# The second expert product in quarters of the output columns, each combined and stored while the next one is made, and half a weight place loaded a tile sooner

## What is computed

```python
h = x @ w_in                                   # 3072 x 2048
g = (a0 + a1*h + a2*h**2 + a3*h**3) / (1 + |b0|*|h| + |b1|*h**2 + 1e-6)
x = g @ w_out                                  # 3072 x 512

logits = x @ phi                               # 3072 x 32
d = softmax(logits, over the tokens)
slot_input = d.T @ x                           # 8 experts x 4 slots x 512
for e in range(8):
    h = np.maximum(slot_input[e] @ w1[e], 0.0) # 4 x 1024
    slot_out[e] = h @ w2[e]                    # 4 x 512
c = softmax(logits, over the slots)
out = c @ slot_out                             # 3072 x 512
```

## Time and profile before

| | |
|---|---|
| median of 3 runs | 519.40 us (519.39 to 519.45) |
| profiled execution | 519.27 us, span 517.5 us |
| busy share of the span: PE, DVE, ACT | 97%, 85%, 77% |
| DMA | 85.3 MB, of it 6.29 MB written |
| chain that ended last | PE 92%, ACT 2%, DMA 2%, DVE 1% |

### The profile page before, as it was taken

How to read it: one execution, slowest core, us unless ns; L and a number is a source line. 1 busy time by engine, 2 the same in 40 slices (tenths; PEclk the granted TensorE clock), 3 DMA queues, 4 the chain that set the end, 5 groups by cost and what they waited for, 6 DMA issues and landing times.

```text
span 517.5 us, 15763 instructions
## 1 busy us (share of the span) xinstructions
PE 503.0 (97%) x6568; PEld 380.1 (73%) x6568; DVE 441.0 (85%) x821; ACT 399.0 (77%) x776; POOL 0.2 (0%) x4
## 2 busy tenths in 40 slices
PE   8899999999999999999999999999999999999993
PEld 7667777877787787778778777877877787654552
DVE  4898999999999999999999999999999999951133
ACT  2877989888888988888898888889888988921122
POOL 0000000000000000000000000000000000000000
PEclk9999999999999999999999999999999999999997
DMA  8982275366313122311313232131322214999998
GB/s 343 418 355 98 90 267 196 95 243 229 119 64 105 42 91 75 97 51 63 104 44 93 72 80 68 63 104 44 100 66 72 75 43 141 424 420 408 417 365 348
DMA packets 18934, 85.29 MB, mean 165 GB/s; under 512 B 2096, under 2 KB 2224, under 8 KB 13488
## 3 DMA queue, kind: packets, MB, share of 16 engines
q1 hardware_dynamic: 18720, 84.09, 44.2%
q10 hardware_dynamic: 144, 0.20, 0.1%
HBM read 77.99 MB, written 6.29 MB: 163 GB/s over the span
## 4 chain that ended last, share of the span: by engine, by line
PE 92%; ACT 2%; DMA 2%; DVE 1%; issue 1%; SPq 0%; DVEq 0%; ACTq 0%
PE hb L425 17%; PE hb L427 17%; PE hb L426 17%; PE gb L355 10%; PE sl L472 4%; PE at L355 4%; PE mb L449 4%; PE at L402 4%; PE at L378 3%; DMA g<-w_in 2%; PE at L615 1%; PE hb L615 1%; PE hb L652 1%; PE mb L457 1%; PE mb L355 1%; PE hb L361 1%
## 5 line engine op out<-in xcount | busy, mean ns | idle before, releaser
L425 PE MATMUL hb<-w_hi,x_hi 128*128 128x512 f32 x384 | 160.2, 417 | 0.8 <-DVE x_lo L955 0.8
L427 PE MATMUL hb<-w_hi,x_lo 128*128 128x512 f32 x384 | 151.7, 395 | 0.0
L426 PE MATMUL hb<-w_lo,x_hi 128*128 128x512 f32 x384 | 151.4, 394 | 0.0
L742 ACT ACTIVATE hs<-hb 128x512 f32<-128x512 f32 x96 | 57.2, 596 | 44.3 <-PE hb L427 44.3
L427 PEld LDWEIGHTS hb<-w_hi,x_lo 128*128 128x128 f32 x384 | 72.1, 188 | 17.7
L425 PEld LDWEIGHTS hb<-w_hi,x_hi 128*128 128x128 f32 x384 | 72.2, 188 | 15.0 <-issue 2.0
L426 PEld LDWEIGHTS hb<-w_lo,x_hi 128*128 128x128 f32 x384 | 72.4, 189 | 12.9
L964 DVE SCALAR_TENSOR_TENSOR h<-h,few,ab 128x512 f32<-128x512 f32 x96 | 71.9, 749 | 10.2 <-ACT h L746 9.9
L751 ACT ACTIVATE h<-h,few 128x512 f32<-128x512 f32 x96 | 70.1, 730 | 9.1 <-DVE h L964 9.1
L969 DVE SCALAR_TENSOR_TENSOR tt<-tt,cst,hs 128x512 f32<-128x512 f32 x96 | 72.2, 752 | 3.4
L979 DVE SCALAR_TENSOR_TENSOR g<-tt,cst,h 128x512 f32<-128x512 f32 x96 | 71.4, 746 | 2.3 <-ACT h L755 0.2
(11 more groups left out here) (154 smaller groups left out, 540.4 us busy)
## 6 DMA issues: line engine op xcount, KB each, us to landing
place<-w SPq DMA_DIRECT2D x27, 1024.0 KB, 9.6
v_in<-v_windows SPq DMA_DIRECT2D x24, 520.0 KB, 3.7
kw<-k_windows SPq DMA_DIRECT2D x24, 512.0 KB, 4.6
qT<-q_t SPq DMA_DIRECT2D x24, 256.0 KB, 2.8
place<-w SPq DMA_DIRECT2D x10, 512.0 KB, 16.6
wout<-w_out_t SPq DMA_DIRECT2D x4, 1024.0 KB, 14.6
wout<-w_out SPq DMA_DIRECT2D x4, 1024.0 KB, 9.0
g<-w_in SPq DMA_DIRECT2D x3, 1024.0 KB, 10.3
```

Source lines behind the costliest of these rows:

```text
L425: mm(o, x_hi[:, p, xs], w_hi[:, f, kd, :], start=kd == 0, stop=False)
L426: mm(o, x_hi[:, p, xs], w_lo[:, f, kd, :], start=False, stop=False)
L427: i = mm(o, x_lo[:, p, xs], w_hi[:, f, kd, :], start=False, stop=kd == KD - 1)
```

## The change

The second product is cut in quarters of 128 output columns instead of halves of 256. A stage of w2 is now one quarter for one group of experts with the whole hidden dimension, 32 matmuls of 128 columns; the order of the stages is quarter 0 and 1 of the first group, 0 and 1 of the second, then quarters 2 and 3 (`W2_STAGES`). The host lays out w2 and the output accordingly. `combine(quarter, part)` makes 16 tiles (part 0: banks of four tiles, 512 columns) or 8 (part 1: banks of two tiles, 256 columns), with matmuls of 128 columns and five banks throughout. Each part has one store, of 1 MB or of 512 KB, from places `o_0` to `o_3` that lie where stages 5 to 7 of w1 were.

`x_hi` and `x_lo` become one buffer `x`, in which the two parts of a tile lie together, so that the part of the even tiles is 4 KB in one piece. The first half of a place of stage 8 is put there, and loaded when the hidden product of tile 22 is done, ahead of the w1 loads that wait for tile 23.

```diff
-        x_hi = sb("x_hi", [P, 2, KD * P], f32r)
-        x_lo = sb("x_lo", [P, 2, KD * P], f32r)
+        x = sb("x", [P, 2, 2, KD * P], f32r)
...
+        x_hi, x_lo = x[:, :, 0, :], x[:, :, 1, :]
...
-        pairs += [in_att + QB * ATT, in_g, in_tmp, in_wout, in_wout + 2 * QB, (in_tmp + 2 * QB, in_wout + 7 * QB)]
+        pairs += [(in_att + QB * ATT, in_att + QB * (ATT + 1)), in_g, in_tmp, in_wout, in_wout + 2 * QB, (in_tmp + 2 * QB, in_wout + 7 * QB)]
...
-        HC = DM // 2
+        HC = DM // 4
+        W2_STAGES = ((0, 0), (1, 0), (0, 1), (1, 1), (2, 0), (2, 1), (3, 0), (3, 1))
+        SETS = ((0, 1), (2,))
...
-        o_bank = [at[:, 0, :], at[:, 1, :], gb[:, :], at[:, 2, :], sl[:, :], hb[:, 0, :], hb[:, 1, :]]
-        o_banks = (5, 7)
+        o_banks = [at[:, 0, :], at[:, 1, :], gb[:, :], hb[:, 0, :], hb[:, 1, :]]
...
-        y_bank = [[at[:, 2, :], sl[:, :]], [hb[:, 0, :], hb[:, 1, :]]]
+        y_bank = [at[:, 2, :], sl[:, :]]
...
             load_pair(3, 1)
+            sp.wait_ge(h_psum, (N - 1) * FC)
+            load_half(8, 0)
             for f in range(FC):
                 sp.wait_ge(h_psum, (N - 1) * FC + f + 1)
                 load_pair(4 + f, 0)
                 load_pair(4 + f, 1)
-            load_pair(8, 0)
+            load_half(8, 1)
...
+            for quarter in range(4):
+                for part in range(2):
+                    cs = slice(16 * HC * part, 16 * HC + 8 * HC * part)
+                    sp.wait_ge(o_dve, 4 * quarter + 2 * part + 2)
+                    sp.wait_ge(o_act, 4 * quarter + 2 * part + 2)
+                    sp.dma_start(out[quarter, :, cs], o_place[quarter][:, cs]).then_inc(stored, 16)
...
+            def combine(quarter, part):
+                cs = slice(HC * quarter, HC * quarter + HC)
+                if part == 0:
+                    pe.wait_ge(s_kept, quarter + 1)
...
+                k = 0
+                for a in SETS[part]:
+                    for m in range(2):
+                        for r in range(4):
+                            u = o_use(quarter, part, r) - len(o_banks)
+                            if k == 0 and u >= 0:
+                                pe.wait_ge((o_dve, o_act)[u % 2], u // 2 + 1)
+                            rows = slice(NS * r, NS * r + NS)
+                            i = mm(o_bank(quarter, part, r)[:, HC * k:HC * k + HC], cT[rows, 2 * a + m, :], s_rows[rows, cs],
+                                   start=True, stop=True)
+                            if k == 2 * len(SETS[part]) - 1:
+                                i.then_inc(o_psums, 1)
+                        k += 1
...
+            expert_out(0)
             expert_turns(1)
-            for stage in range(9, 13):
-                expert_out(stage)
-            expert_out(13, (0, 1))
+            expert_out(1)
+            expert_out(2)
+            expert_out(3, (0,))
             slot_rows(0)
-            expert_out(13, (2, 3))
+            expert_out(3, (1,))
             combine(0, 0)
-            expert_out(14)
+            slot_rows(1)
+            expert_out(4, (0,))
             combine(0, 1)
-            expert_out(15, (0, 1))
-            combine(0, 2)
-            expert_out(15, (2, 3))
-            slot_rows(1)
-            for a in range(PAIRS // 4):
-                combine(1, a)
+            expert_out(4, (1,))
+            combine(1, 0)
+            expert_out(5, (0,))
+            combine(1, 1)
+            expert_out(5, (1,))
+            expert_out(6, (0,))
+            slot_rows(2)
+            expert_out(6, (1,))
+            combine(2, 0)
+            expert_out(7, (0,))
+            combine(2, 1)
+            expert_out(7, (1,))
+            slot_rows(3)
+            combine(3, 0)
+            combine(3, 1)
```

More of the change, by code:

```diff
@@ L270, in load_pair, with load_half @@
                                  ).then_inc(last_ready if part else stage_ready[stage], 16)
+            def load_half(stage, half):
+                sp.dma_start(place(stage, half), (w1[half // 2, stage] if stage < 4 else w2_of(stage, half // 2))
+                             [:, QUARTER * (half % 2):QUARTER * (half % 2) + QUARTER]).then_inc(stage_ready[stage], 16)
             def load_qk(n):
@@ L310, in _ @@
             sp.wait_ge(sc_psum, N)
[L311 removed]
+            load_half(3, 1)
             sp.wait_ge(o_psum, N)
@@ L337, in _ @@
                     load_pair(15, x, part_of)
[L339 to L346, removed]
+            for quarter in range(4):
[4 more added lines that the diff above has]
+                    sp.dma_start(out[quarter, :, cs], o_place[quarter][:, cs]).then_inc(stored, 16)
+            sp.wait_ge(stored, 16 * 8)
         @block.tensor
@@ L638, in combine_turns @@
                 i.then_inc(cT_psum, 1)
[L640 to L649, removed]
-                        pe.wait_ge(last_ready, 32)
[L651 to L660, removed]
-                mm(mb[:, cs], srep[:, :], so[:, cs], start=True, stop=True).then_inc(rep_psum, 1)
[L663 to L667, removed]
+            def expert_out(i, halves=(0, 1)):
+                quarter, grp = W2_STAGES[i]
+                stage = 8 + i
+                for half in halves:
+                    if half == 0:
+                        pe.wait_ge(stage_ready[stage], 32 if stage == 15 else 16 * landings(stage))
+                    elif stage == 15:
+                        pe.wait_ge(last_ready, 32)
+                    if quarter == 0:
+                        pe.wait_ge((hT_act, hT_dve)[half], grp + 1)
+                    for j in range(4):
+                        ft = 4 * half + j
+                        for c in range(4):
+                            u = mm(y_bank[quarter % 2][NS * c:NS * c + NS, HC * grp:HC * grp + HC], hT[grp][:, ft, NS * c:NS * c + NS],
+                                   place(stage, c // 2 * 2 + half)[:, HC * (4 * (c % 2) + j):HC * (4 * (c % 2) + j) + HC],
+                                   start=ft == 0, stop=ft == FET - 1)
+                if half == 1:
+                    u.then_inc(stage_used, 1)
@@ new lines, in slot_rows @@
+            def slot_rows(quarter):
+                cs = slice(HC * quarter, HC * quarter + HC)
+                pe.wait_ge(y_sb, 2 * quarter + 2)
+                if quarter == 0:
+                    pe.wait_ge(hT_dve, 2)
+                    pe.wait_ge(cT_dve, 1)
+                mm(mb[:, cs], srep[:, :], so[:, cs], start=True, stop=True).then_inc(rep_psum, 1)
+            def combine(quarter, part):
+                cs = slice(HC * quarter, HC * quarter + HC)
+                if part == 0:
+                    pe.wait_ge(s_kept, quarter + 1)
+                if quarter == 0 and part == 0:
@@ L908, in _, with rows_copy, evict @@
                     A(cT[:, 0:4, :].rearrange("p a b -> p (a b)"), gb[:, :], ACT.Copy).then_inc(cT_act, 1)
-            for ch in range(2):
-                cs = slice(HC * ch, HC * ch + HC)
-                act.wait_ge(rep_psum, ch + 1)
+            def rows_copy(quarter):
+                cs = slice(HC * quarter, HC * quarter + HC)
+                act.wait_ge(rep_psum, quarter + 1)
                 A(s_rows[:, cs], mb[:, cs], ACT.Copy).then_inc(s_kept, 1)
[L913 to L916, removed]
+            def evict(quarter, part):
+                w = 2 * HC * len(SETS[part])
+                for r in (1, 3):
+                    act.wait_ge(o_psums, o_use(quarter, part, r) + 1)
+                    A(o_out(quarter, part, r), o_bank(quarter, part, r)[:, 0:w], ACT.Copy).then_inc(o_act, 1)
+            rows_copy(0)
+            evict(0, 0)
+            rows_copy(1)
+            evict(0, 1)
+            evict(1, 0)
+            evict(1, 1)
+            for quarter in (2, 3):
+                rows_copy(quarter)
+                evict(quarter, 0)
+                evict(quarter, 1)
         @block.vector
```

83 lines of the change are left out of this document (41 added, 42 removed).

## The result

| | before | changed |
|---|---|---|
| median | 519.39 us (519.35 to 519.45) | 522.39 us (522.13 to 523.15) |
| ratio | | 1.0060, 95% interval 1.0046 to 1.0073 |
| profiled execution, span | 519.27, 517.5 us | 522.13, 520.4 us |
| end of the last expert stage on PE | 503.9 | 510.5 (forecast 507.7) |
| issue of the first store of the last group | 507.99 | 514.82 (forecast 512.1) |

What follows compares the result with a forecast made beforehand. The prediction took PE's chain, then the store drain, to set the end: 3.8 us more on PE, a drain 3.9 shorter, the end moving about 0.1 us. It forecast 519.5 us, range 517.4 to 522.0.

Steps and rivals of the forecast that it cites:

- The bound: End of the kernel: PE's way to the last expert stage, the chain to the first stores, then the drain.
- (a): Second expert product on PE: twice as many matmuls of 128 columns, half the size at half the price, cost 0.
- rival A: Combines on PE: weight loads no longer hide, slower, mostly 520.6 to 522.5 us, up to 524.4; chance 0.2.
- (b): PE's returns to the expert product from other matmuls: 0.13 us each, eight instead of four, +0.5.
- (c): Combines before the last expert stage's end: six calls at 0.11 us a set, 5.3 us instead of 3.6.
- (e): Replicating matmuls on PE: three of 0.42 us instead of one of 0.63, plus 0.2 slot-sum wait, together +0.8.
- (d): Bank waits in the second parts of quarters 1 and 2: 0.42 us each, together +0.8.
- The sum: PE's terms up to the end of the last expert stage: +3.8 us, ending at 507.7 instead of 503.9.
- From the last stage to the store: Chain from the last stage's end to the last quarter's first store: 4.4 us, issue at 512.1.
- The drain of 3.9 us: Last quarter's stores: 1.57 MB at 403 GB/s, 3.9 us, a drain 3.9 us shorter than before.
- The early half place: A 512 KB load moved to the end of tile 22's hidden product: cost 0, gain 0.
- Rival B: DMA queue: stores fill its holes if PE's pieces are cheaper, faster, mostly 517.0 to 518.4 us; chance 0.25.

Runs made afterwards that it cites:

- experiment 1: Changed kernel with 32 tiny matmuls at PE's start in place of four filling ones (112 records more net): 523.63 us.
- experiment 2: Kernel before with every matmul of the second expert product cut in two of 128 columns: 524.15 us.
- experiment 3: Changed kernel without the loads of stages 11 to 15 and PE's waits for them, so the output is not the layer's: 519.58 us.
- experiment 8: Changed kernel with the first half of the columns in halves, combine(2, 1) behind the last half stage, quarter 3's first store in two pieces: 519.25 us.
- experiment 9: Kernel before with its third combine behind the last half stage and DVE's slot sum ahead of that combine's copies: 519.34 us.
- experiment 10: experiment 9 with the early half place and the first half's stores in pieces of 512 KB: 518.56 us, 0.9983 of the kernel before.
- experiment 4: Changed kernel with 16 tiny matmuls (64 more PE records) at the start, nothing taken away: 527.65 us.
- experiment 5: Changed kernel without the early half place, the 512 KB of stage 8 loaded behind the four w1 stages again: 522.58 us.
- experiment 7: Changed kernel with combine(2, 1) behind the last half stage and the last slot sum ahead of DVE's copies of it: 521.98 us.

## Why the prediction was wrong

**The bound** was read right: a queue with holes, PE's chain behind them. Every store but the last group's is off the path, before and after.

**(a) The expert product at half the size and half the price**, a cost of 0, is the step that failed. The price of a record was right: 64 of them take 1.86 us where 32 of twice the size take 1.84. What I took from the logits is a burst of 32 weight loads and 32 matmuls in 0.88 us, a quarter of a block; it says nothing of a stream that stays as dense for 15 us while the loads fill the queue. There the instructions themselves come too late: two stops that cost 3.0 us, where nothing was forecast. They show up in the combines, since that is where the blocks end in this kernel; of the five near the experts in experiments 1 and 2, four lie in the expert product. I had named it in half a sentence of rival A ("PE fed late with its doubled number of instructions") and given it no price, though the profile's page had what it takes: 52 fetches for 13,136 records, and a full queue beside the experts. The measured 522.39 lies in A's "520.6 to 522.5", but those figures were worked out for slow weight loads: that is luck.

**(b), (c), (e)** came out within 0.1: returns at 0.13, a set at 0.11, a first part without a stop at 1.10 to 1.11, a replicating matmul at 0.42; of the 0.2 of waiting for the slot sum in (e) less than 0.1 is there. Rival A, loads that no longer hide, falls with the 0.11.
**(d)** Two bank waits of 0.4 were forecast. Quarter 2's second part takes 1.05 (508.46 to 509.51), against 0.66 without a wait: 0.4, as forecast. Quarter 1's takes 0.87 (502.10 to 502.97), a wait of 0.2. Together 0.6, not 0.8. In experiment 3, where no stop delays PE just before, both parts take 1.06, which is the forecast 0.8.

**The sum** on PE was +3.8. From 483.99 to the end of the last stage the kernel before takes 19.9 us. Without loads (experiment 3) the changed order takes 508.0 - 484.20 = 23.8, so +3.9; with them 510.5 - 483.87 = 26.6, +6.7. The 2.8 between these runs are the two combines with a stop (3.04 and 2.21, against 1.10 and 1.11 in experiment 3: 3.0 more) less 0.2 of the bank wait in (d). It is also the difference of the times, 522.39 - 519.58. From the last stage to the store I had 4.4; it is 4.3 (510.5 to 514.82). The drain of 3.9 us was right.

**The early half place** at nothing was right, on both sides.

**Rival B** (the queue sets the end) is not what this change meets; but experiments 8 and 9 show that it stands directly behind: as soon as the last group starts 1 us earlier, the queue takes over.

**The range** ended at 522.0 since I let A reach 522.5 in words and cut it at 522.0. With what only the result showed, a stop priced as the difference between a fetch's way (6.2 us at most) and a block of 4.6, and the product and combines of the quarters three such blocks long, the range would have reached 519.5 + 3 x 1.6 = 524.3.

## What to carry to other kernels

Cutting matmuls in half keeps PE's time only while its instructions arrive. Count records per microsecond over a whole fetched block, not over a burst, and compare the time of a block with the way of a fetch beside the loads of that stretch. An idle piece with no releaser, in the middle of a group of equal matmuls, is looked for at equal distances in the count of instructions before it is put down to the code around it. And where PE and the queue end within a microsecond of each other, look at both: here a shorter PE chain alone bought nothing (experiment 9), and the only gain came with earlier stores beside it (experiment 10).

## What the hardware showed that I had not expected

- PE stops at the ends of blocks of about 256 records: after 12957, 13210, 13465 and 13720 in one run. The fetch behind a block's start began 0.3 us after it with the data queue empty (experiment 3), 1.3 to 3.8 with it full, by the count of records. Each of the 13 stops of 0.4 us and more without a releaser, in six traces, ends 1.2 to 1.6 us after the end of a fetch.
- Where the blocks are cut matters, and so do edits far from the place: without useless records at the start the changed kernel takes 522.4 us, with 112 more 523.6, with 64 more 527.7, mostly through a stop of 3.0 us at 126 us, some 360 us before the second expert product.
- Stops of 2.1 us (experiment 2) and of 1.6 us (4 and 5) were followed by a granted clock of 0.50 for 3 us or so; the changed kernel's own stop of 1.57 was not, nor were experiment 7's of 1.1 and 1.2. What decides between them is open.
- A queue that had been full for 9 us ended with one or two DMA engines at work 1.7 us longer than the rest (experiment 8).
